# Two fused feed-forward blocks on one core: the first product of each block as seven block products instead of eight, and each block over all tokens in turn

## What is computed

```python
qn = q / (np.linalg.norm(q, axis=1, keepdims=True) + 1e-06)      # q, k, v: (1, 6016, 256)
kn = k / (np.linalg.norm(k, axis=1, keepdims=True) + 1e-06)
s = kn.transpose(0, 2, 1) @ qn / tau                             # 256 x 256
a = softmax(s)                                                   # over the last axis
x = (v @ a).reshape(6016, 256)
h = x @ w_in;  x2  = (h - np.tanh(h)) @ w_out                     # block one, d_ff = 2048
h = x2 @ w_in2; out = np.where(h > 0, h, np.exp(np.minimum(h, 0)) - 1) @ w_out2   # block two
```

## Time and profile before

| | |
|---|---|
| runs | 1094.79, 1095.77, 1095.93 us; median 1095.77 us |
| profiled execution | 1094.33 us, of which 1092.5 us are the span of the trace |
| TensorE busy | 1083.3 us, 4908 matmul passes |
| VectorE busy | 708.0 us |
| ScalarE busy | 536.1 us |
| granted TensorE clock | 1.000 of full speed |

### The profile page before, as it was taken

One profiled execution on the slowest core, in us unless ns is written; L12 is line 12 of the kernel. 1 busy time (PEld: TensorE's weight loads), 2 busy tenths in 40 slices (PEclk: granted clock), 3 DMA queues, 4 the chain that ended last, 5 costly groups with the idle time before them and its releaser, 6 DMA issues.

```text
span 1092.5 us, 14169 instructions
## 1 busy us (share of the span) xinstructions
PE 1083.3 (99%) x4908; PEld 907.8 (83%) x4908; DVE 708.0 (65%) x1139; ACT 536.1 (49%) x893; POOL 0.8 (0%) x7
## 2 busy tenths in 40 slices
PE   8999999999999999999999999999999999999998
PEld 7887888888888888888888888888888888888898
DVE  5886666666665766666666666666576666666565
ACT  6675545444444544544544544444454454444443
POOL 0000000000000000000000000000000000000000
PEclk9999999999999999999999999999999999999999
DMA  9941010110100101101011011010010010000010
GB/s 355 324 120 20 1 20 0 20 20 1 20 6 15 20 0 19 19 0 19 0 19 19 0 19 19 0 19 13 6 19 0 14 19 0 0 14 7 1 20 15
DMA packets 106237, 33.42 MB, mean 31 GB/s; under 512 B 96864, under 2 KB 101344, under 8 KB 105952
## 3 DMA queue, kind: packets, MB, share of 16 engines
q1 hardware_dynamic: 105776, 32.13, 11.7%
q10 hardware_dynamic: 432, 0.92, 0.2%
HBM read 26.87 MB, written 6.16 MB: 30 GB/s over the span
## 4 chain that ended last, share of the span: by engine, by line
PE 97%; DVE 1%; ACT 0%; DMA 0%; issue 0%; ACTq 0%
PE h_ps L375 15%; PE h_ps L377 15%; PE h_ps L376 15%; PE x_ps L375 8%; PE x_ps L376 8%; PE x_ps L377 8%; PE out_ps L375 8%; PE out_ps L376 8%; PE out_ps L377 8%; PE x_ps L383 4%; DMA q_ring<-q_dram 0%; DVE g_lo L710 0%; DVE wf_lo L740 0%; DVE w_out_lo L710 0%; DVE g L845 0%; ACT g_hi L651 0%
## 5 line engine op out<-in xcount | busy, mean ns | idle before, releaser
L710 DVE TENSOR_TENSOR g_lo<-g,g_hi 128x512 fp32r<-128x512 f32 (+1 forms) x384 | 261.4, 681 | 224.9 <-ACT g_hi L651 116.5
L651 ACT ACTIVATE g_hi<-g 128x512 fp32r<-128x512 f32 (+1 forms) x192 | 119.5, 622 | 205.5 <-DVE g L845 205.1
L637 ACT ACTIVATE g_hi<-g 128x512 fp32r<-128x512 f32 (+1 forms) x192 | 119.7, 624 | 131.7 <-PE x_ps L377 70.3
L644 ACT ACTIVATE g<-h_ps 128x512 f32<-128x512 f32 (+1 forms) x192 | 113.0, 588 | 137.2 <-PE h_ps L377 136.3
L826 DVE TENSOR_TENSOR g<-h_ps,g 128x512 f32<-128x512 f32 (+1 forms) x192 | 129.6, 675 | 30.2 <-ACT g L630 30.1
L375 PE MATMUL x_ps<-g_hi,w_out_hi 128*128 128x512 f32 (+1 forms) x384 | 148.1, 386 | 0.2 <-DVE g_lo L710 0.2
L377 PE MATMUL h_ps<-x_hi,w_in_lo 128*128 128x512 f32 (+1 forms) x384 | 148.2, 386 | 0.0
L377 PE MATMUL h_ps<-vT_hi,wf_lo 128*128 128x512 f32 (+1 forms) x384 | 148.1, 386 | 0.0
L375 PE MATMUL h_ps<-x_hi,w_in_hi 128*128 128x512 f32 (+1 forms) x384 | 148.0, 385 | 0.1
L375 PE MATMUL h_ps<-vT_hi,wf_hi 128*128 128x512 f32 (+1 forms) x384 | 148.0, 385 | 0.1
L376 PE MATMUL h_ps<-x_lo,w_in_hi 128*128 128x512 f32 (+1 forms) x384 | 147.9, 385 | 0.0
(11 more groups left out here) (105 smaller groups left out, 1091.1 us busy)
## 6 DMA issues: line engine op xcount, KB each, us to landing
v_blocks<-v_dram SPq DMA_DIRECT2D x88, 64.0 KB, 2.2
out_dram<-out_sb SPq DMA_DIRECT2D x88, 64.0 KB, 1.8
k_ring<-k_dram SPq DMA_DIRECT2D x9, 512.0 KB, 10.0
q_ring<-q_dram SPq DMA_DIRECT2D x9, 512.0 KB, 10.8
stage_a<-moe_w_in_dram SPq DMA_DIRECT2D x4, 512.0 KB, 8.3
stage_b<-moe_w_out_dram SPq DMA_DIRECT2D x1, 2048.0 KB, 8.7
w_in_raw<-moe_w_in_dram SPq DMA_DIRECT2D x1, 2048.0 KB, 10.8
stage_a<-moe_w_out_dram SPq DMA_DIRECT2D x1, 2048.0 KB, 8.6
```

Source lines behind the costliest of these rows:

```text
L637: nc.scalar.activation(g1_hi[i % 2][:, 0:n], g1[i % 2][:, 0:n], ACT.Copy).then_inc(g1_rounded, 1)
L644: nc.scalar.activation(g2[i % 2][:, 0:n], h2_ps[i % 2][:, 0:n], ACT.Exp).then_inc(exp2_ready, 1)
L651: nc.scalar.activation(g2_hi[i % 2][:, 0:n], g2[i % 2][:, 0:n], ACT.Copy).then_inc(g2_rounded, 1)
L710: return nc.vector.tensor_tensor(lo, x, hi.bitcast(F32), ALU.subtract)
```

## The change

The hidden channels are taken two units at a time (a "quad", 8 in a block), and the tokens in pairs of equal halves (`WIDTH`: five pairs of 2 x 512 tokens and one of 2 x 448, 6 pairs). The first product of one quad and one pair is then a 2 x 2 by 2 x 2 block product: channel halves by units, and channel halves by token halves. It is computed in Winograd's form with seven products P1 to P7 instead of eight. Each is `three_passes` over one combined weight block (`w_ops`, seven blocks per quad: A11, A12, A22, and the sums S1 to S4) and one combined activation block (`t_hi`, `t_lo`: V11, V21, V22 and the four differences T). The sums of products are formed in PSUM where they can be: P1 lies in bank X, ScalarE copies X into bank Y and P2 accumulates on it (h11); P6 accumulates on X, ScalarE copies X into Z and P7 accumulates on that; P3 accumulates on X. P5 goes into bank Q and is copied to SBUF by ScalarE (`h12`). VectorE adds it to Z (h22) and to X (h12); P4 accumulates on Z (h21). The second product stays as it was, 24 passes for the same work, into four banks R.

The program is a row of 96 steps (`ALL`): block one for all six pairs, eight quads each, then block two for all six. x2 leaves block one through ScalarE (`move_x2`, into `side`) to a DRAM buffer `x2_scratch`, and is loaded again by `load_x2` for block two. `w_in2` and `w_out2` are loaded, summed, rounded and split during the last steps of block one and the first of block two, step by step into the place of block one's weights. The output leaves by `turn_out` on VectorE (a 32 x 32 block transpose out of PSUM, as before) and 16 DMAs per pair. `wf` is made in plain float32, one pass over `w_in1` per half of the channels instead of three fp32r passes, four of its eight pieces after the first products have begun. Block two's h11 and h21 take their `exp` low part with a second ScalarE instruction (`Relu` of 1 - e) and one `scalar_tensor_tensor` on VectorE, h12 and h22 as before.

TensorE's order, and what it waits for:

```diff
+            def product(n, op, ps, start):
+                p, u, width, part = place(n)
+                if u == 0:
+                    pe.wait_ge(t_split, ops_split(p, op))
+                if p in (0, PAIRS):
+                    pe.wait_ge(w_split, QUADS * part + u + 1)
+                return three_passes(ps[:, 0:width], w_ops[:, HI, u, op, :], w_ops[:, LO, u, op, :],
+                                    t_hi[p % 2][:, op, 0:width], t_lo[p % 2][:, op, 0:width], start, True)
...
+            def second(n, b):
...
+                pe.wait_ge(g_split[b], n + 1)
+                if first:
+                    wait(pe, r_moved[j], CC * p)
+                if p in (0, PAIRS) and b == "11":
+                    pe.wait_ge(w_out_split, QUADS * part + u + 1)
...
+            def between(n, i):
+                if n == 0:
+                    if i < 2:
+                        wf_product(WF_EARLY + 2 * i)
+                        wf_product(WF_EARLY + 2 * i + 1)
                     return
...
+                order = ("11", "22", "21", "12") if n % QUADS == 0 else ("11", "22", "12", "21")
+                second(n - 1, order[i])
+            for n in range(ALL):
+                wait(pe, g_ready["12"], n)
+                product(n, P1, X, True).then_inc(p1_done, 1)
+                wait(pe, p5_copied, n)
+                product(n, P5, Q, True).then_inc(p5_done, 1)
+                between(n, 0)
+                pe.wait_ge(y_seeded, n + 1)
+                product(n, P6, X, False).then_inc(p6_done, 1)
+                product(n, P2, Y, False).then_inc(h_ready["11"], 1)
+                between(n, 1)
+                pe.wait_ge(z_seeded, n + 1)
+                product(n, P7, Z, False).then_inc(p7_done, 1)
+                product(n, P3, X, False).then_inc(p3_done, 1)
+                between(n, 2)
+                pe.wait_ge(h_ready["22"], n + 1)
+                product(n, P4, Z, False).then_inc(h_ready["21"], 1)
+                between(n, 3)
+            for i in range(4):
+                between(ALL, i)
```

ScalarE's and VectorE's order in a step:

```diff
+                act.wait_ge(p1_done, n + 1)
+                wait(act, g_ready["11"], n)
+                copy_bank(Y, X, n, y_seeded)
+                if n > 0:
+                    round_g(n - 1, "21")
...
+                act.wait_ge(p5_done, n + 1)
+                wait(act, g_ready["12"], n)
+                copy_bank(h12, Q, n, p5_copied)
...
+                act.wait_ge(p6_done, n + 1)
+                wait(act, g_ready["21"], n)
+                copy_bank(Z, X, n, z_seeded)
+                low(n, "11", Y)
...
+                round_g(n, "11")
...
+                if n + 1 < QUADS:
+                    round_w(n + 1)
+                if n < QUADS:
+                    round_w_out(n)
...
+                low(n, "22", h22)
+                low(n, "12", h12)
+                if moves and u == 0:
+                    move_x2(p - 1, 0, 0)
+                    move_x2(p - 1, 1, 0)
+                round_g(n, "22")
+                low(n, "21", Z)
+                round_g(n, "12")
+            round_g(ALL - 1, "21")
...
+                if n > 0:
+                    form_g(n - 1, "21", Z)
+                    split_g(n - 1, "12")
+                if moves and u == 1:
+                    turn_out(p - PAIRS - 1, 0, 1)
+                    turn_out(p - PAIRS - 1, 1, 1)
+                if n > 0:
+                    split_g(n - 1, "21")
+                if n + 1 < QUADS:
+                    sum_w(n + 1)
...
+                    if u == 3:
+                        form_t(p + 1, P5)
+                        split_t(p + 1, P1)
+                    if u == 4:
+                        split_t(p + 1, P2)
+                        split_t(p + 1, P5)
+                        form_t(p + 1, P6)
...
+                form_g(n, "11", Y)
+                dve.wait_ge(p7_done, n + 1)
+                dve.wait_ge(p5_copied, n + 1)
+                nc.vector.tensor_tensor(h22[:, 0:width], Z[:, 0:width], h12[:, 0:width], ALU.add).then_inc(h_ready["22"], 1)
+                dve.wait_ge(p3_done, n + 1)
+                nc.vector.tensor_tensor(h12[:, 0:width], X[:, 0:width], h12[:, 0:width], ALU.add).then_inc(h_ready["12"], 1)
+                split_g(n, "11")
+                if n < QUADS:
+                    split_w_out(n)
+                if moves and u == 0:
+                    turn_out(p - PAIRS - 1, 0, 0)
+                    turn_out(p - PAIRS - 1, 1, 0)
+                if part == 1:
+                    elu_low(n, "22")
+                    elu_low(n, "12")
+                form_g(n, "22", h22)
+                form_g(n, "12", h12)
+                if n + 1 < QUADS:
+                    split_w(n + 1)
+                split_g(n, "22")
```

SyncE: the order of the loads at the start, and of those at the change of blocks:

```diff
-            w_in1_rows = w_in1.rearrange("(a p) f -> p a f", p=P)
-            for g in range(GROUPS):
-                sp.dma_start(stage_a[:, g * CC * 512:(g + 1) * CC * 512].rearrange("p (a f) -> p a f", a=CC),
-                             w_in1_rows[:, :, g * 512:(g + 1) * 512]).then_inc(loaded_w_in1[g], 16)
...
             load_v(0)
...
+            sp.dma_start(w_in1_sb[:, :, :], w_in1.rearrange("(a p) f -> p a f", p=P)).then_inc(loaded_w_in1, 16)
+            sp.dma_start(w_out_raw[:, :, :], w_out1.rearrange("(u p) c -> p u c", p=P)).then_inc(loaded_w_out1, 16)
+            sp.wait_ge(vt_ready, 4)
             load_v(1)
...
+            def load_w_in2(u):
+                sp.wait_ge(h_ready["21"], FIRST2 - QUADS + u + 1)
+                cols = slice(2 * u * P, 2 * (u + 1) * P)
+                sp.dma_start(w_raw[:, :, u, 0, :], w_in2[0:P, cols].rearrange("p (s f) -> p s f", s=2)).then_inc(loaded_w_in2[u % 2], 16)
+                sp.dma_start(w_raw[:, LO, u, 1:3, :], w_in2[P:C, cols].rearrange("p (s f) -> p s f", s=2)).then_inc(loaded_w_in2[u % 2], 16)
...
+            for p in range(PAIRS - 1):
+                if p > 0:
+                    store_x2(p - 1)
+                if p + 2 < PAIRS:
+                    sp.wait_ge(vt_ready, 4 * (p + 2))
+                    load_v(p + 2)
+            load_x2(0)
+            store_x2(PAIRS - 2)
+            for u in range(QUADS):
+                load_w_in2(u)
+                if u > 0:
+                    load_w_out2(u - 1)
+            load_x2(1)
+            load_w_out2(QUADS - 1)
+            store_x2(PAIRS - 1)
```

More of the change, by code:

```diff
@@ L45 @@
 GROUPS = F // 512
-UNITS_PER_GROUP = UNITS // GROUPS
-PIECES = 8
-PIECE = CC * F // PIECES
-UNITS_PER_PIECE = UNITS // PIECES
+TILE = 512
+WIDTH = [512] * 5 + [448]
+PAIRS = len(WIDTH)
+TOKEN0 = [2 * sum(WIDTH[:p]) for p in range(PAIRS)]
+QUADS = UNITS // 2
+ALL = 2 * PAIRS * QUADS
+FIRST2 = PAIRS * QUADS
+assert 2 * sum(WIDTH) == N
+P1, P2, P4, P3, P5, P6, P7 = range(7)
+A11, A12, A22, S4, S1, S2, S3 = range(7)
+OPS = 7
+READY = {P1: 1, P2: 2, P5: 3, P3: 4, P6: 5, P4: 6, P7: 7}
 CHUNKS = [2, 2, 3] + [4] * 9 + [2, 2]
@@ L362, in _ @@
+            for p in range(PAIRS - 1):
+                if p + 2 < PAIRS:
+                    load_x2(p + 2)
+                store_out(p)
+            store_out(PAIRS - 1)
+            sp.wait_ge(out_stored, 16 * PAIRS * 4 * (P // BLOCK))
         @block.gpsimd
@@ L909, in _, with form_g @@
-            iterations(dve, iteration)
+            split_t(0, P1)
+            split_t(0, P2)
+            split_t(0, P5)
+            form_t(0, P6)
+            split_t(0, P3)
+            split_t(0, P6)
+            form_t(0, P4)
+            form_t(0, P7)
+            split_t(0, P4)
+            sum_w(0)
+            split_t(0, P7)
+            split_w(0)
+            def form_g(n, b, src):
+                p, u, width, part = place(n)
+                dve.wait_ge(low_ready[b], n + 1)
+                h, to = src[:, 0:width], g[b][:, 0:width]
+                if part == 0:
+                    nc.vector.tensor_tensor(to, h, to, ALU.subtract).then_inc(g_ready[b], 1)
+                elif b in ("12", "22"):
+                    dve.wait_ge(low_step[b], n - FIRST2 + 1)
+                    nc.vector.tensor_tensor(to, h, to, ALU.max).then_inc(g_ready[b], 1)
+                else:
+                    nc.vector.scalar_tensor_tensor(out=to, in0=to, scalar=-1.0, in1=h, op0=ALU.mult, op1=ALU.max).then_inc(g_ready[b], 1)
@@ L913 @@
+            form_g(ALL - 1, "21", Z)
+            split_g(ALL - 1, "12")
+            split_g(ALL - 1, "21")
+            for j in range(2):
+                for m in range(CC):
+                    turn_out(PAIRS - 1, m, j)
 INPUTS = ["q", "k", "v", "tau", "moe_w_in", "moe_w_out", "moe2_w_in", "moe2_w_out"]
```

856 lines of the change are left out of this document (344 added, 512 removed), and 5 rows, old and new, of the table V_SLOT.

## The result

The changed kernel takes 1083.0 us (median of four runs, 1082.5 to 1084.3), the kernel before 1095.6: a ratio of 0.9888, with a 95% interval of 0.9871 to 0.9905. That is 12.6 us less, where 25 were forecast (1070.5). The profiled execution has a span of 1080.9 us against the 1067.2 of the forecast's sum, so 13.7 us have to be found.

What follows compares the result with a forecast made beforehand. TensorE's number of passes was taken as the bound. 63.0 us before step 0, 960.5 of passes, and the waits and leaving summed to a 1067.2 us span, giving 1070.5 us; range 1052 to 1096.

Steps and rivals of the forecast that it cites:

- Block two's ring through `form_g`: Block two: VectorE's chain from P3 to the next P1 ends too late, 0.15 us per step, 48 steps, 7.2 us.
- The transposes: Block two's output: two transposes at the first step of pairs 2 to 6, 5 x 1.2 = 6.0 us.
- The bank copies: ScalarE's PSUM-to-PSUM copies: no row, taken at 0.60 us; the one to Y may cost 1.0 before TensorE waits.
- Rivals 1 and 2: Rival 1: waits vanish, 1045 to 1060, 0.14; rival 2: ring behind P3 longer, 1083 to 1093 at 0.10, past turning 0.12.
- block one's cover: Block one: VectorE's chain ends before the next P1 needs it, with 0.6 us to spare, so it is hidden.
- After the last pass: 0.43, transpose 0.7, four issues, landing: 4.2.: Kernel's end: time from the last pass through output transpose, four DMA issues and landing, 4.2 us.
- Together 7.5: Steps 41 to 48: waits while block two's weights are prepared, including 2.2 for late w_in2, 7.5 us rounded up.
- Rival 3, the clock (0.06): TensorE runs at half speed for one step behind gaps before steps 0 and 1, adding 10 us: 1081; chance 0.06.
- The steps with weights in them: Steps 1 to 6 of block one: P1 of the next step waits for split_w, 1.05 us each, 6.3 in all.

Runs made afterwards that it cites:

- experiment 6: Changed kernel with unread VectorE instructions added behind the split of g11, one or two a step in steps 35 to 39, one in steps 64 to 71: 1088.5 us.
- Experiment 1: Changed kernel with the last pair's sixteen stores split, eight on ScalarE's queue and eight on SyncE's: 1080.5 us.
- experiment 2: Changed kernel with SyncE issuing load_w_in2(0) between the two halves of store_x2(4), not behind both: 1078.0 us.
- Experiment 7: Changed kernel with P1 waiting for the sum h12 of the step before, no longer for form_g "12": 1073.3 us.
- experiment 11: Block two's weight splits moved behind form_g "12" on VectorE, atop P1-wait, VectorE-order, two-queue-store, early-w_in2 and pre-step-0 matmul edits: 1052.1 us.
- experiment 3: Changed kernel with unread TensorE work added in two gaps, three matmuls before step 0 and twelve passes before step 1: 1078.1 us.
- experiment 8: On the changed kernel with P1 waiting for h12's sum: split_w (steps 0 to 6) moved ahead of form_g "22" and "12", output transposes behind form_g "12": 1060.4 us.

## Why the forecast was wrong

The direction and the places were right, half of the size was not. Against its own steps:

**Right.** Passes of 512 are 0.227 us apart and 45 to a step. Block one has no wait (10.20, all of steps 8 to 38). Block two's ring through `form_g` costs 0.15 to 0.18 a step against 0.15, and each instruction added to it its full pitch (experiment 6). The transposes cost 1.17 each time against 1.2. The bank copies, priced at 0.60 with no row, take 0.57, and additions on PSUM 0.68. Rivals 1 and 2 fall: no wait vanished, and the ring is at most 0.1 us longer than laid out (block one's cover of 0.5 us).

**"After the last pass: 0.43, transpose 0.7, four issues, landing: 4.2."** This is the step that failed most plainly: 8.8 from the modelled end of that pass. The changed kernel stores the last pair in sixteen DMAs, of which two can go out before the last pass starts, and the queue needs 8.16 us. I had counted four, as if the others were out by then. Experiment 1 shows it: with the issues on two queues 2.5 us go.

**"Together 7.5" for steps 41 to 48.** Measured 13.4. I had seen that `load_w_in2(0)` stands behind `store_x2(4)` and priced it at 2.2. It cost 3.1 of wait and then 1.2 of clock, all gone in experiment 2. Another 3.0 us of the miss lie in steps 43 to 49, which took 8.3 us over their passes where I had 4.85 and a rounding. The wait of P4 for h22 in steps 44 and 45 (0.99 us in each) I had left out, and took only P1's, and step 49, 1.03 over its passes, I had left out whole. The last 0.8 is the price of a pass of 448 columns, 0.2027 and not 0.2006. Experiment 7 got 1.3 us of these waits back and experiment 11 another 1.4; the rest was not taken apart.

**Rival 3, the clock (0.06).** It was real, and the sum had nothing for it. I had set it aside since the one idle stretch of the trace, 4.7 us at the start, seemed to be followed by full speed. That was misread: the first passes behind it start 0.427 us apart and the later ones 0.216. My 0.226 for a pass (36.15 / 160) is a mean over both. The trace of the kernel before bore the rule out. I had forecast two gaps of 2 to 4 us and there are three; each costs 1.0 to 1.9 us, where the rival had 10 for both. The Trainium skill ("TensorE: Matmul & The Clock Gate", Part 1, What's actually happening) describes a throttled default that activity lifts, and these traces agree: 1.2 GHz behind the first gap of every profile and behind most of the long ones, 2.4 after some us of passes, full behind the two gaps that were filled with work (experiment 3).

**"The steps with weights in them", 1.05 each.** Steps 2 to 6 took 1.15 to 1.77 over their passes, step 1 2.56 with half a clock in it. The mechanism, `split_w` at the end of the chain, was right (experiment 8 moves it, and steps 2 and 3 go to 10.2), and the term was too small.

**What offset it.** `v` landed at 41.8 and not 45.5, which gave 1.5 us back. It was not the whole 3.7, since VectorE then stood at 43.6 waiting for ScalarE's root, which hangs on TensorE's work on q and k. That these 14 passes at half speed are what made the root late is likely, and not shown.

Summed: end 4.6, hand-over 5.9 (1.2 of it clock), steps 0 and 1 with the clock and steps 2 to 7 4.3, block two 1.0, less 1.5 and 0.9. What stays open is the 0.2067 us pitch of 448 columns, in two kernels throughout the end and in single steps of others, and how the waits of steps 43 to 49 divide.
